# Attention and two feed-forward layers on one core: slot order, result copies between exponentials, a root by Newton steps, later weight loads

## The reference

```python
def _attn_ref(q, k, v):                        # (4, 8, 576, 64) each
    scores = scale * np.matmul(q, k.transpose(0, 1, 3, 2))
    rel = pos[:, None] - pos[None, :]
    scores = np.where((rel >= 0) & (rel < 64), scores, -1000000000.0)
    attn = np.exp(scores - np.max(scores, axis=-1, keepdims=True))
    attn = attn / (np.sum(attn, axis=-1, keepdims=True) + 1e-09)
    return np.matmul(attn, v)
def _moe_ref(x, w_gate, w_val, w_out, rms_g):  # 512 -> 1536 -> 512
    rms = np.sqrt(np.mean(x * x, axis=-1, keepdims=True) + 1e-06)
    xn = x / rms * rms_g
    g = xn @ w_gate
    return g * (1.0 / (1.0 + np.exp(-g))) * (xn @ w_val) @ w_out
def _moe2_ref(x, w_in, w_out):                 # 512 -> 2048 -> 512
    r = np.maximum(x @ w_in, 0.0)
    return (r * r) @ w_out
```

## Time and profile before

| | |
|---|---|
| median of 3 runs | 884.71 us (882.9 to 884.73) |
| the profiled execution's own time | 882.57 us |
| its span | 880.8 us |
| TensorE busy in it | 864.2 us (98%) |
| VectorE, ScalarE, GpSimd busy | 546.8, 468.2, 541.8 us |
| mean granted TensorE clock | 0.994 |

### The profile page before, as it was taken

How to read it: one execution, slowest core, us unless ns; L and a number is a source line. 1 busy time by engine, 2 the same in 40 slices (tenths; PEclk the granted TensorE clock), 3 DMA queues, 4 the chain that set the end, 5 groups by cost and what they waited for, 6 DMA issues and landing times.

```text
span 880.8 us, 16629 instructions
## 1 busy us (share of the span) xinstructions
PE 864.2 (98%) x6436; PEld 852.2 (97%) x6436; DVE 546.8 (62%) x617; ACT 468.2 (53%) x990; POOL 541.8 (62%) x521
## 2 busy tenths in 40 slices
PE   7898999999999999999999999999999999999998
PEld 6687999999999999999999999999999999999998
DVE  4759676558567548755557677676477674577222
ACT  5877665645565644555555455444455443554332
POOL 3746398583589665388856368563386743585332
PEclk9989999999999999999999999999999999999999
DMA  8863122222222212222222222222422222420222
GB/s 277 264 205 100 49 73 72 61 61 60 84 73 72 67 54 60 78 73 73 73 65 60 72 73 73 60 60 71 146 72 73 60 60 61 153 75 26 54 66 96
DMA packets 87007, 75.01 MB, mean 85 GB/s; under 512 B 5520, under 2 KB 70032, under 8 KB 86928
## 3 DMA queue, kind: packets, MB, share of 16 engines
q1 hardware_dynamic: 86784, 73.65, 28.1%
q10 hardware_dynamic: 144, 0.29, 0.1%
HBM read 69.21 MB, written 4.72 MB: 84 GB/s over the span
## 4 chain that ended last, share of the span: by engine, by line
PE 94%; DVE 3%; ACT 1%; issue 1%; POOL 1%; DVEq 0%; POOLq 0%
PE banks L732 30%; PE banks L734 30%; PE banks L733 30%; PE banks L691 1%; PE banks L633 1%; ACT probs L1004 1%; DVE probsT L1244 1%; PE banks L705 1%; DVE acts L1184 0%; PE banks L665 0%; DVE banks L1224 0%; PE banks L641 0%; DVE neg_max L1231 0%; PE banks L713 0%; PE banks L697 0%
## 5 line engine op out<-in xcount | busy, mean ns | idle before, releaser
L732 PE MATMUL banks<-xc_hi,w_hi 128*128 128x384 f32 x844 | 282.7, 335 | 0.2 <-DVE xc_lo L1216 0.2
L734 PE MATMUL banks<-xc_hi,w_lo 128*128 128x384 f32 x844 | 281.9, 334 | 0.0
L733 PE MATMUL banks<-xc_lo,w_hi 128*128 128x384 f32 x844 | 281.9, 334 | 0.0
L584 POOL TENSOR_TENSOR d_lo<-d_raw,d_hi 128x512 fp32r<-128x512 f32 x84 | 127.3, 1516 | 174.8 <-ACT d_hi L935 174.8
L732 PE MATMUL banks<-hs_hi,d_hi 128*128 128x384 f32 x672 | 225.1, 335 | 0.1
L734 PE MATMUL banks<-hs_hi,d_lo 128*128 128x384 f32 x672 | 224.5, 334 | 0.0
L733 PE MATMUL banks<-hs_lo,d_hi 128*128 128x384 f32 x672 | 224.5, 334 | 0.0
L1322 DVE TENSOR_TENSOR hs_lo<-h,hs_hi 128x768 fp32r<-128x768 f32 x84 | 86.4, 1028 | 137.4 <-ACT hs_hi L935 137.2
L732 PEld LDWEIGHTS banks<-xc_hi,w_hi 128*128 128x128 f32 x844 | 158.5, 188 | 0.6 <-DVE xc_lo L1216 0.4
L733 PEld LDWEIGHTS banks<-xc_lo,w_hi 128*128 128x128 f32 x844 | 158.5, 188 | 0.0
L734 PEld LDWEIGHTS banks<-xc_hi,w_lo 128*128 128x128 f32 x844 | 158.4, 188 | 0.0
(11 more groups left out here) (93 smaller groups left out, 1074.5 us busy)
## 6 DMA issues: line engine op xcount, KB each, us to landing
d_raw<-in_w_down SPq DMA_DIRECT2D x48, 256.0 KB, 2.6
w_raw<-in_w_gate SPq DMA_DIRECT2D x36, 256.0 KB, 2.9
w_raw<-in_w_val SPq DMA_DIRECT2D x72, 128.0 KB, 2.8
d_raw<-in_w_out SPq DMA_DIRECT2D x36, 256.0 KB, 2.6
v_sb<-in_v_rows SPq DMA_DIRECT2D x16, 384.0 KB, 5.0
w_raw<-in_w_in SPq DMA_DIRECT2D x24, 256.0 KB, 2.7
w_raw<-in_w_in SPq DMA_DIRECT2D x48, 128.0 KB, 2.7
q_sb<-in_qT SPq DMA_DIRECT2D x16, 288.0 KB, 4.7
```

The lines of the kernel that those rows point to most:

```text
L584: nc.gpsimd.tensor_tensor(d_lo[m % 2][:], d_raw[m % 2][:], d_hi[m % 2][:].bitcast(F32), ALU.subtract).then_inc(dlo_done, 1)
L732: pe.matmul(ps, w_h, v_h, start=first, stop=False, skip_group_check=joined)
L733: pe.matmul(ps, w_h, v_l, start=False, stop=False, skip_group_check=joined)
L734: return pe.matmul(ps, w_l, v_h, start=False, stop=last, skip_group_check=joined)
```

## The change

- The slot order on TensorE becomes scores, transposes of g-2, values of g-3.
- On ScalarE the result copies of group g-3 move from ahead of the eight exponentials to between the fourth and the fifth.
- The root and the inverse (an activation and a reciprocal) give way to a first guess by integer arithmetic on the bits and two Newton steps on VectorE, seven instructions of 128 x 6 elements, each waiting for the one before (`inverse_root`). In slot 13 they stand, with the mean square, ahead of VectorE's masked copy; in the runs they stand in step 8. GpSimd's diagonals read `guess`.
- The two halves of squares that ScalarE computed move to VectorE's queue, in slot 11.
- The loads of the first two blocks of weights move from behind sequences 1 and 3 in SP's queue to behind 6 and 8, those of the first two `d` blocks from behind 9 and 10 to behind 10 and 11; GpSimd's splits of them move to later slots.
- The constant `ones` is set first on GpSimd; TensorE begins with nine products on `ones` where it had six on `ident`.

```diff
@@ -46,7 +47,7 @@
 MASKED = -1e9 / SCALE
-PICK, CONSTS = 8, 14
+PICK, CONSTS = 8, 13
@@ -62,7 +63,10 @@
 HELD = 6
-WARM = 6
+WARM = 9
+ROOT_SEED = float(0x5F1FFFF9)
+ROOT_STEPS = ((-0.703952253, 0.703952253 * 2.38924456), (-0.5, 1.5))
+STEPS = 1 + 3 * len(ROOT_STEPS)
@@ -172,6 +176,8 @@
         rms = sb("rms", [P, TB], F32)
+        guess = sb("guess", [P, TB], F32)
+        resid = sb("resid", [P, TB], F32)
         assert top[0] <= nc.sbuf_usable_end, (top[0], nc.sbuf_usable_end)
@@ -212,6 +218,7 @@
         consts = sem("consts")
+        ones_set = sem("ones_set")
         gain_in = sem("gain_in")
@@ -240,7 +247,7 @@
         sq_done, sq_sum, ms_mm, ms_done = sem("sq_done"), sem("sq_sum"), sem("ms_mm"), sem("ms_done")
-        rms_done, rinv_done, diag_done = sem("rms_done"), sem("rinv_done"), sem("diag_done")
+        rinv_done, diag_done = sem("rinv_done"), sem("diag_done")
         rb_first = sem("rb_first")
@@ -407,10 +414,10 @@
                     load_v(i + 1)
-                if i in (1, 3):
-                    load_w((i - 1) // 2)
-                if i in (9, 10):
-                    load_d(i - 9)
+                if i in (6, 8):
+                    load_w((i - 6) // 2)
+                if i in (10, 11):
+                    load_d(i - 10)
@@ -429,6 +436,7 @@
         def _(pool):
+            nc.gpsimd.memset(ones[:], 1.0).then_inc(ones_set, 1)
             nc.gpsimd.memset(ident[:], 0.0).then_inc(consts, 1)
@@ -455,8 +463,6 @@
                                             channel_multiplier=-sign).then_inc(consts, 1)
-            pool.wait_ge(consts, step)
-            nc.gpsimd.memset(ones[:], 1.0).then_inc(consts, 1)
             pool.wait_ge(consts, CONSTS)
@@ -480,11 +486,11 @@
-                pool.wait_ge(rinv_done, q + 1)
+                pool.wait_ge(rinv_done, STEPS * (q + 1))
                 pool.wait_ge(ms_mm, q + 1)
...
                                         ident[:].unsqueeze(1).broadcast_to([P, TB, P]),
-                                        rms[:].unsqueeze(2).broadcast_to([P, TB, P]), ALU.mult).then_inc(diag_done, 1)
+                                        guess[:].unsqueeze(2).broadcast_to([P, TB, P]), ALU.mult).then_inc(diag_done, 1)
@@ -528,29 +534,29 @@
                                             by_unit(sums[:, n % PR, :]), ALU.mult).then_inc(scaled, 1)
-                if g == 5:
-                    high1_plain(0)
-                if g == 6:
-                    low1_plain(0)
-                if g == 7:
-                    high2_plain(0)
-                    low2_plain(0)
                 if g in (8, 9):
...
                 if g == 10:
-                    high1_plain(1)
-                    high2_plain(1)
+                    high1_plain(0)
                 if g == 11:
...
                     square_half(1, 1)
+                if g == 12:
+                    low1_plain(0)
                 if g == 13:
...
                 if g == 14:
+                    high2_plain(0)
+                    low2_plain(0)
+                if g == 15:
+                    high1_plain(1)
+                    high2_plain(1)
+                if g == 16:
                     low1_plain(1)
-                if g == 15:
+                if g == 17:
                     low2_plain(1)
@@ -636,9 +642,10 @@
                     if g == 0:
+                        pe.wait_ge(ones_set, 1)
+                        for n in range(WARM):
+                            pe.matmul(bank[5][:, 0:P], ones[:], ones[:], start=True, stop=True)
                         pe.wait_ge(consts, 6)
-                        for n in range(WARM):
-                            pe.matmul(bank[5][:, 0:P], ident[:], ident[:], start=True, stop=True)
                         pe.wait_ge(first_in, 32)
@@ -654,8 +661,6 @@
                     mm.then_inc(qk_done, 1)
-                if 0 <= g - PV_LAG < GROUPS:
-                    value_product(g - PV_LAG)
                 if 0 <= g - T_LAG < GROUPS:
@@ -665,6 +670,8 @@
                     mm.then_inc(tr_done, 1)
+                if 0 <= g - PV_LAG < GROUPS:
+                    value_product(g - PV_LAG)
@@ -750,7 +757,6 @@
                 if g == 10:
-                    pe.wait_ge(consts, CONSTS)
                     pe.wait_ge(sq_pool, KT)
@@ -951,17 +957,14 @@
-            def square_half(k, c):
-                cols = slice(c * NT, (c + 1) * NT)
-                nc.scalar.activation(squares[0][k][:, cols], half_cols(0, k, c), ACT.Square).then_inc(sq_done, 1)
+            def exponential(g, u):
+                return nc.scalar.activation(probs[g % PR][:, u % UNITS, u // UNITS, :],
+                                            s_ps[g % 2][:, u * P:u * P + WIN], ACT.Exp,
+                                            bias=neg_max[:, g % PR, u:u + 1], scale=SCALE,
+                                            accum_out=sums[:, g % PR, u:u + 1])
...
-
-            def root(q):
-
-                act.wait_ge(ms_done, q + 1)
-                nc.scalar.activation(rms[:], rms[:], ACT.Sqrt).then_inc(rms_done, 1)
@@ -990,6 +993,12 @@
             for g in range(TAIL):
+                if g < GROUPS:
+                    act.wait_ge(biased, g + 1)
+                    if g >= PR:
+                        act.wait_ge(tr_done, g - PR + 1)
+                    for u in range(UNITS):
+                        exponential(g, u)
                 if 0 <= g - O_LAG < GROUPS:
@@ -997,20 +1006,9 @@
                 if g < GROUPS:
-                    act.wait_ge(biased, g + 1)
-                    if g >= PR:
-                        act.wait_ge(tr_done, g - PR + 1)
-                    for u in range(GU):
-                        mm = nc.scalar.activation(probs[g % PR][:, u % UNITS, u // UNITS, :], s_ps[g % 2][:, u * P:u * P + WIN], ACT.Exp,
-                                                  bias=neg_max[:, g % PR, u:u + 1], scale=SCALE,
-                                                  accum_out=sums[:, g % PR, u:u + 1])
+                    for u in range(UNITS, GU):
+                        mm = exponential(g, u)
                     mm.then_inc(exp_done, 1)
-                if g == B_GROUP + O_LAG:
-                    act.wait_ge(o_out, O_DONE[B_GROUP + 1])
-                    square_half(2, 1)
-                    square_half(3, 1)
-                if g == 12:
-                    root(0)
                 if g in (15, 16):
@@ -1109,8 +1107,6 @@
                             square(r + 1, s - 2)
-                        if s == 8:
-                            root(r + 1)
                         if s == 11:
@@ -1175,10 +1171,21 @@
-            def inverse(q):
-
-                dve.wait_ge(rms_done, q + 1)
-                nc.vector.reciprocal(rms[:], rms[:]).then_inc(rinv_done, 1)
+            def inverse_root(q):
+
+                done = STEPS * q
+                dve.wait_ge(ms_done, q + 1)
+                nc.vector.tensor_scalar(guess[:].bitcast(I32), rms[:].bitcast(I32), -0.5, ROOT_SEED, ALU.mult,
+                                        ALU.add).then_inc(rinv_done, 1)
+                for n, (by, plus) in enumerate(ROOT_STEPS):
+                    dve.wait_ge(rinv_done, done + 1 + 3 * n)
+                    nc.vector.tensor_tensor(resid[:], guess[:], guess[:], ALU.mult).then_inc(rinv_done, 1)
+                    dve.wait_ge(rinv_done, done + 2 + 3 * n)
+                    nc.vector.scalar_tensor_tensor(out=resid[:], in0=resid[:], scalar=by, in1=rms[:], op0=ALU.mult,
+                                                   op1=ALU.mult).then_inc(rinv_done, 1)
+                    dve.wait_ge(rinv_done, done + 3 + 3 * n)
+                    nc.vector.scalar_tensor_tensor(out=guess[:], in0=resid[:], scalar=plus, in1=guess[:], op0=ALU.add,
+                                                   op1=ALU.mult).then_inc(rinv_done, 1)
@@ -1234,6 +1241,9 @@
                     nc.vector.reciprocal(sums[:, n % PR, :], sums[:, n % PR, :]).then_inc(inverted, 1)
+                if g == 13:
+                    mean_square(0, bank[5])
+                    inverse_root(0)
                 if 0 <= g - T_LAG < GROUPS:
@@ -1246,10 +1256,11 @@
                         ALU.mult).then_inc(pt_out, 1)
-                if g == 12:
-                    mean_square(0, bank[5])
-                if g == 13:
-                    inverse(0)
+                if g == 11:
+                    dve.wait_ge(o_out, O_DONE[B_GROUP + 1])
+                    for k in (2, 3):
+                        of = half_cols(0, k, 1)
+                        nc.vector.tensor_tensor(squares[0][k][:, NT:PW], of, of, ALU.mult).then_inc(sq_done, 1)
                 if g in (14, 15):
@@ -1334,8 +1345,7 @@
                         mean_square(r + 1, v_banks(r)[0])
-                    if s == 9 and r + 1 < PAIRS:
-                        inverse(r + 1)
+                        inverse_root(r + 1)
                     dve.wait_ge(p2_done, n)
```

More of the change, by code:

```diff
@@ L30 @@
 BF16 = mybir.dt.bfloat16
+I32 = mybir.dt.int32
 ALU = mybir.AluOpType
```

## The result

The changed kernel is slower: median 886.94 us of 20 runs against 882.95 us of 20 runs of the kernel before, ratio 1.0047 with a 95% interval of 1.0032 to 1.0062, so +4.1 us (2.8 to 5.5). The forecast was 882.4, faster. The median of before is 882.95 over 20 runs, where the three shown ahead had 884.71. One run of each kernel was slow (1070.12 us after, 1963.76 before) and stands in the medians but not in the ratio.

What follows compares the result with a forecast made beforehand. TensorE was taken as the bound, its 800.0 us stream of products fixed and only its start movable; attention terms summed to -1.8 us, 880.8 on the profiled 882.57, and with 1.6 carried 882.4, range 879.0 to 886.5.

Steps and rivals of the forecast that it cites:

- whose readers have over 1 us: nothing: Large layers, step 8: the root ahead of ga, va and vb on VectorE costs nothing, as their readers have slack.
- A small one is 0.18: VectorE: a small instruction takes 0.18 us plus 0.03 hand-over, so seven root instructions take 1.5 us, plus 0.2.
- rival (B): Whole kernel: copies, low clock in slots 11 to 13 and a dear root cancel the gain, 884.7 us; chance 0.33.
- -1.8 (the reload): Attention, slots 11 to 13: 1.8 us of the time put down to the Exp table reload after the root's swap.
- +1.4 (slot 13): Attention, slot 13 to 14: root and mean square ahead of VectorE's masked copy lengthen 3.15 to 4.55 us.
- 2 x 0.5 us that I called hidden: Slot 11: squares on VectorE delay slot 12 some 1.0 us, hidden because slot 13 waits for TensorE.
- Slot 10 to 11: Attention: the step from slot 10 to 11, with the first sums of squares, takes 4.95 us for 5.43, -0.5.
- Rival (C): TensorE's clock: from three more low-clock slots the change costs +4, turning -1.8 into +2, 887 us; chance 0.15.
- the floor of 3.70: Attention: the shortest slot period rises from 3.15 to 3.70 us, as copies between exponentials add about 0.55.
- they end 0.8 us ahead of T(g): Attention, transposes first: values end 0.8 us before slot g's first exponential, T(g), giving their result copy 2 us of slack.
- Slots 11 to 13: Attention: 9.25 us for 12.65 between first exponentials of these slots, -3.4 at the higher clock, -1.8 at the lower.
- The carry of 1.6 us: Final sum: 1.6 of the 2.1 us between profiled time and median of the runs shown, added to 880.8.

Runs made afterwards that it cites:

- the PSUM run: The changed kernel with the Newton root's mean square and residual in PSUM, so no root instruction reads two SBUF operands, places in the queue unchanged: 1.0012 of the kernel before.

## Why the prediction was wrong

**The step that failed is the price of the root by Newton steps, and most of all "whose readers have over 1 us: nothing"**, the large layers. It stood on "A small one is 0.18", read on a reciprocal with one operand while GpSimd was idle. The seven instructions took 3.3 us and not 1.5, and TensorE lost 1.12 us twice. I had named this case and put it inside rival (B) at no price. Moving the root out of the way gave 1.7 us back; giving it a PSUM operand, or ScalarE, gave 3.1 and 3.3 back. For the root as a whole I had -1.8 (the reload) and +1.4 (slot 13), and alone on the kernel before it measured +3.2. That is 3.6 of the 5.9 us between the -1.8 forecast and the +4.1 measured.

The cause is shown by the PSUM run: the instructions of the chain with their inputs in SBUF ended only when the GpSimd instruction under way had ended, and those with an input in PSUM did not wait for it. The other way round, GpSimd's squares took 2.30 us beside VectorE's and 1.61 without them. The page "SBUF — State Buffer" of the Trainium skill (SBUF: two separate sides) has this as an exclusive lock on a shared port pair, for a VectorE operation in a two-port mode, or with two SBUF inputs against a GpSimd operation that reads SBUF. The traces agree for the instructions with two SBUF inputs, with 0.59 to 0.98 us for 0.17; the first guess (0.79 us) has one, and no trace shows its mode. I had not weighed it.

**Root in slot 13**: +1.4 forecast, +1.75 measured, inside the bounds (+1.0 to +2.6), partly by luck. Without the held instruction the slot takes 4.15 us (the PSUM run), 0.4 less than my 4.55; the hold adds 0.75, which I had not counted.

**Squares on VectorE**: the 2 x 0.5 us that I called hidden were not, because they lengthened GpSimd's squares by 0.7 us, and the sums wait for these. On ScalarE they would have held the sums nearly as long (3.9 us behind T(11) for 4.2). By the one profiled execution of each; in time it isn't resolved.

**Slot 10 to 11**: -0.5 forecast, +1.0 measured. My chain was for the higher clock; after, the clock is 0.57 from 46 to 50 us. Rival (C) named the low clock as deciding; it rose from 10 to 18 us in the profiled runs. But over the 19 runs in the ratio the mean granted clock is 0.9908, and over those of the kernel before beside the experiments 0.9918 to 0.9921. That is 16 against 14 us at the lower level, and as this level is half the speed, I estimate 1 us of the loss at most. With the root alone the clock is 0.9913 and the loss 3.2 us. So (C)'s 887 was met in number only: it was a change of +2 counted from 884.71, and the measured one is +4. Whether the later loads or the longer slots bring the low clock into slot 10 is open: in the profiles of all seven kernels with late loads T(10) to T(11) is 6.3 to 10.4 us at a clock of 0.55 to 0.76, in those of the seven others 5.2 to 7.3 at 0.64 to 1.00, one execution each.

**Copies and order**: the floor of 3.70 was right to 0.01 us, the sum over slots 3 to 10 was 26.15 for 26.1, and the pair alone measured 1.0002. This part of the mechanism held. That the order alone would cost 2.8 us was not in my text, though its reason was half there: "they end 0.8 us ahead of T(g)" holds for the long slot only.

**Slots 11 to 13**: -1.8 to -3.4 forecast, -0.8 measured. Of the 12.65 us before, 1.8 was put down to the table, and the traces give the reload 1.1 to 1.3. The rest of it was low clock in one execution: the other kernels with the reload and values first have 6.35 and 8.23 us from T(12) to T(13) for its 9.02. After, that stretch takes 6.65 at a clock of 0.55, so I take it that what the reload gave back went into the clock and the late sums. In time the reload's worth cannot be told from none.

**The carry of 1.6 us** from the profiled time to the median was a mistake of its own: three runs with a median of 884.71 stood for a kernel whose 20 have 882.95, 0.4 above the profiled one. By luck it brought the forecast nearer to the measured time: without it 880.8 would have stood against 886.94.

The parts add up, within a scatter of over 2 us: root 3.2, order and copies 0.2, loads 0.4, early products -0.4 are 3.4 us, and with the 1.1 of the squares 4.5, for 4.1 measured. Only the first of these is outside its own scatter. Of the stream's 2.7 us, 0.5 is not explained by the two gaps.

## What to carry to other kernels

Price an instruction by a row with the same operands and the same neighbours: here small VectorE instructions on SBUF beside a busy GpSimd cost what was left of GpSimd's instruction, four times of seven in step 8 and once in slot 13; one operand in PSUM freed them. Put such a chain where its queue is idle anyway, not ahead of the instruction that the critical engine reads next. Before an effect of one profiled execution enters a sum, look whether that execution ran at the low clock there, and don't take three runs for the median.

## What the runs showed of the hardware

Eight VectorE instructions of 128 x 6 elements each took 0.17 us with an input in PSUM beside GpSimd at work; with all inputs in SBUF four of the chain of seven took 0.59 to 0.79. The 24 one-column products with 128 x 128 weights took 2.74 us at the higher clock and 5.12 with a granted clock of 0.50. And TensorE stood for 1.74 us (before) and 2.05 us (later loads) without a releaser in the profile, each time within 1 us of the start of a packet of the instruction queue; that the packet is the cause is not shown.
